# A fused mLSTM and two-MLP kernel in fp32: the order of the first three attention units, the weight swap two tiles earlier, and the last tile in thirds

## The reference, cut to what matters

```python
for t in range(S):                       # S = 768, 4 batches, 8 heads, head size 40
    m_new = np.maximum(f_gate[:, :, t] + m, i_gate[:, :, t])
    f_stab = np.exp(f_gate[:, :, t] + m - m_new)
    i_stab = np.exp(i_gate[:, :, t] - m_new)
    C = f_stab * C + i_stab * outer(v[t], k[t]);  n = f_stab * n + i_stab * k[t]
    y[:, :, t] = sigmoid(o_gate[t]) * (C @ q[t]) / np.maximum(np.abs(n @ q[t]), 1.0)
x = y as 3072 tokens x 320
h = x @ w_in;   x = np.maximum(0.01 * h, h) @ w_out      # MLP 1, 320 -> 2048 -> 320
h = x @ w2_in;  out = (h * np.cos(h)) @ w2_out           # MLP 2, same sizes
```

## Time and profile before

| | |
|---|---|
| median of 3 runs | 853.45 us (852.97 to 853.61) |
| profiled execution | 853.69 us, of which span 852.0 us |
| busy in the span: PE, DVE, ACT, POOL | 834.5, 626.1, 475.5, 311.9 us |
| DMA | 76.23 MB, 89 GB/s mean |

### The profile page before, as it was taken

The page is one execution under the profiler, slowest core; times in us unless marked ns, Lnnn a source line. Parts: engine busy times, 40 slices in busy tenths (PEclk is TensorE's granted clock), DMA queues, the critical chain, the costliest instruction groups (busy, mean ns, idle before and its releaser), DMA issues.

```text
span 852.0 us, 15386 instructions
## 1 busy us (share of the span) xinstructions
PE 834.5 (98%) x5618; PEld 820.9 (96%) x5618; DVE 626.1 (73%) x1175; ACT 475.5 (56%) x1041; POOL 311.9 (37%) x343
## 2 busy tenths in 40 slices
PE   7899999999999999999999989999999999999997
PEld 7789999999999999999999989999999999999997
DVE  6689777666676666776663478888888888888885
ACT  4355433433443434334335677777777777777775
POOL 4774533222222232432003663333333333333333
PEclk9899999999999999999999999999999999999999
DMA  8392822323433323225003430302010202020000
GB/s 261 102 299 73 279 91 90 136 90 100 151 132 112 136 90 136 90 90 203 2 27 120 135 110 1 117 1 70 1 71 1 70 1 71 0 70 2 15 10 23
DMA packets 38450, 76.23 MB, mean 89 GB/s; under 512 B 3434, under 2 KB 27498, under 8 KB 38378
## 3 DMA queue, kind: packets, MB, share of 16 engines
q1 hardware_dynamic: 38330, 75.23, 26.7%
q10 hardware_dynamic: 48, 0.05, 0.0%
HBM read 63.28 MB, written 11.99 MB: 88 GB/s over the span
## 4 chain that ended last, share of the span: by engine, by line
PE 58%; issue 23%; POOL 13%; DVE 2%; ACT 1%; DMA 1%; POOLq 0%; SPq 0%; ACTq 0%
PE h L574 22%; POOL g_lo L1283 13%; PE acc L584 7%; PE acc L586 7%; PE acc L585 7%; PE x L551 4%; PE s L497 3%; PE x L558 2%; PE x L539 1%; PE s L525 1%; PE s L574 1%; DMA kvo_s<-kvo 1%; PE acc L654 1%; DVE kvo_s L931 0%; DVE g_lo L1006 0%
## 5 line engine op out<-in xcount | busy, mean ns | idle before, releaser
L574 PE MATMUL h<-xT,w_in 128*128 128x384 f32 x1536 | 304.7, 340 | 1.3 <-DVE xT L998 1.3
L574 PEld LDWEIGHTS h<-xT,w_in 128*128 128x128 f32 x1536 | 268.4, 189 | 1.7 <-DVE xT L998 1.6
L700 ACT ACTIVATE t_f<-h 128x384 f32<-128x384 f32 x192 | 94.2, 490 | 296.0 <-PE h L574 296.0
L584 PE MATMUL acc<-w_out,g_hi 128*128 128x320 f32 x768 | 243.7, 317 | 4.6 <-POOL g_lo L1283 4.6
L586 PE MATMUL acc<-w_out,g_lo 128*128 128x320 f32 x768 | 237.4, 309 | 0.0
L585 PE MATMUL acc<-w_out,g_hi 128*128 128x320 f32 x768 | 236.1, 307 | 0.0
L1283 POOL TENSOR_TENSOR g_lo<-g_f,g_hi 128x384 fp32r<-128x384 f32 x128 | 131.7, 1029 | 213.6 <-ACT g_hi L700 213.6
L584 PEld LDWEIGHTS acc<-w_out,g_hi 128*128 128x128 f32 x768 | 144.4, 188 | 7.3 <-POOL g_lo L1283 3.1
L585 PEld LDWEIGHTS acc<-w_out,g_hi 128*128 128x128 f32 x768 | 144.5, 188 | 0.0
L586 PEld LDWEIGHTS acc<-w_out,g_lo 128*128 128x128 f32 x768 | 144.1, 188 | 0.0
L1013 DVE TENSOR_TENSOR g_f<-h,t_f 128x384 f32<-128x384 f32 x128 | 71.1, 555 | 96.7 <-ACT t_f L700 94.1
(11 more groups left out here) (134 smaller groups left out, 864.0 us busy)
## 6 DMA issues: line engine op xcount, KB each, us to landing
qk_s<-qk SPq DMA_DIRECT2D x24, 512.0 KB, 3.8
kvo_s<-kvo SPq DMA_DIRECT2D x24, 484.0 KB, 6.0
D<-g_dram SPq DMA_DIRECT2D x21, 512.0 KB
x_dram<-stage SPq DMA_DIRECT2D x8, 960.0 KB, 7.9
xT<-x_dram SPq DMA_DIRECT2D x8, 960.0 KB, 5.0
qe<-q SPq DMA_DIRECT2D x24, 180.0 KB, 4.0
out<-x SPq DMA_DIRECT2D x24, 160.0 KB, 1.8
raw_in<-w1i SPq DMA_DIRECT2D x8, 384.0 KB, 4.4
```

The source lines that it names most:

```text
L574: last = nc.tensor.matmul(bank[:, 0:BLOCK], w(a), x[:, k, :], start=(n == 0), stop=(n == 7))
L584: nc.tensor.matmul(acc[t][:, 0:DM], g_hi[:, s, r], w_out[:, 0, j, :], start=(j == 0), stop=False)
L700: copy = lambda o, i, **k: nc.scalar.activation(o, i, ACT.Copy, **k)
```

## The change

It touches the lists ahead of the first tile on all five engines, the place of one weight piece, the swap of the weights and the last tile. The core of the diff:

```diff
-LATE_IN = {0: 2, 2: 3, 5: 4, 7: 5, 9: 6, 11: 7}
+LATE_IN = {2: 2, 3: 3, 5: 4, 7: 5, 9: 6, 11: 7}
-SWAP_IN, SWAP_OUT = LAG, LAG + 1
+SWAP_IN, SWAP_OUT = 1, LAG + 1
-WARM = (9, 2, 3, 3, 4, 3)
+WARM = (10, 2, 5, 6)
...
             sp.wait_ge(G_done, 2)
             store_gates(g_dram, G_s[1].rearrange("p (c t) -> p c t", c=TILES), 1).then_inc(scratch, 16)
-            wait_count(xT_done, 1)
+            wait_count(x1_done, 1)
+            wait_count(U_done, 1)
             load_unit_inputs(0, 3)
             sp.wait_ge(gate_exp, 3)
             store_gates(e_dram, keep[:, TILES:CHUNKS, :], 1).then_inc(scratch, 16)
-            load_raw_in(w1i, 2)
             sp.wait_ge(scratch, 32)
             sp.wait_ge(g_stored, 16)
             load_unit_decays(0, 3)
+            load_raw_in(w1i, 2)
...
             warm_up(WARM[0], acc[0])
-            unit_scores(0, 0)
-            warm_up(WARM[1], acc[0])
             pe.wait_ge(sel_done, 2)
             pe.wait_ge(G_done, 1)
             spread_decays(0, 0)
             pe.wait_ge(i_step, 2)
             turn_columns(i_s, 0, 0)
             spread_decays(0, 1)
+            unit_scores(0, 0)
...
             spread_decays(1, 1)
+            spread_decays(2, 0)
             pe.wait_ge(cols_done, 2)
             unit_within(0, 0)
             unit_state(0, 0)
-            spread_decays(2, 0)
             spread_decays(2, 1)
-            warm_up(WARM[2], s_bank[1])
-            pe.wait_ge(dx_done, 2 * TILES)
             unit_scores(0, 2)
+            unit_state(0, 1)
+            pe.wait_ge(dx_done, 4)
             unit_carried(0, 1)
             unit_within(0, 1)
-            warm_up(WARM[3], s_bank[1])
+            pe.wait_ge(dx_done, 2 * TILES)
+            warm_up(WARM[1], acc[2])
             unit_transpose(0, 0)
-            unit_state(0, 1)
-            warm_up(WARM[4], h_bank[1])
             unit_carried(0, 2)
             unit_within(0, 2)
             unit_state(0, 2)
-            warm_up(WARM[3], h_bank[1])
             unit_transpose(0, 1)
-            warm_up(WARM[5], acc[2])
+            warm_up(WARM[2], acc[2])
             unit_transpose(0, 2)
+            warm_up(WARM[3], acc[2])
...
+            act.wait_ge(consts, 2)
+            copy(sel[:, :, :], ident[:, 0:HEADS].unsqueeze(2).to_broadcast([P, HEADS, CHUNK])).then_inc(sel_done, 1)
+            gate_scale(0)
             sigmoid_exp(0, 0)
-            gate_scale(0)
...
+            gate_maxima(1)
             sigmoid(0, 0)
-            gate_maxima(1)
             first_probs(0)
             sigmoid(0, 1)
-            first_probs(1)
+            first_probs(1, (0,))
+            gate_decays(1)
+            first_probs(1, (1,))
             outputs(0, 0)
-            first_probs(2)
+            first_probs(2, (0,))
+            sigmoid(0, 2)
+            first_probs(2, (1,))
             state(0, 1)
             outputs(0, 1)
-            gate_decays(1)
             x_lo(0, 0, xT[:, 0])
-            sigmoid(0, 2)
             outputs(0, 2)
...
+                if i >= 1 and ends(row, i - 1):
+                    last_cosines(row, i - 1)
...
+                elif ends(row, i):
+                    last_reduction(row, i, 0)
...
+                last_reduction(row, i, 1)
+                product(0)
+                last_reduction(row, i, 2)
+                rest(0)
+                product(1)
+                rest(1)
+                product(2)
+                rest(2)
```

More of the change, by code:

```diff
@@ L275, in swapped @@
             def swapped(self, i, after):
-                j = i - after
-                return j if self.starts(BLOCKS - 1, 0) and 0 <= j < FT else None
+                j = self.tile(i) - (BLOCKS - 1) * FT - after
+                return j if 0 <= j < FT else None
             def turn2(self, i):
@@ L304, in build, with ends, thirds @@
         TILES_TOTAL = 2 * BLOCKS * FT
+        def ends(row, i):
+            return isinstance(row.first, int) and row.tile(i) == TILES_TOTAL - 1
+        def thirds(x):
+            return [(c, x[:, c * P:(c + 1) * P]) for c in range(TILES)]
         def exists(row, i):
@@ L475, in score_banks @@
         def score_banks(b, c):
-            return (s_bank, h_bank, acc[1:3])[c] if first(b, c) else s_bank
+            return h_bank if first(b, c) and c == 1 else s_bank
         def output_bank(b, c):
@@ L481, in turn_bank @@
         def turn_bank(b, c):
-            return score_banks(b, c)[1] if first(b, c) else x_bank
+            return (acc[1], h_bank[1], s_bank[1])[c] if first(b, c) else x_bank
         @block.tensor
@@ L581, in second_product @@
                     r = slice(t * P, (t + 1) * P)
+                    if ends(row, i) and t > 0:
+                        pe.wait_ge(lo_done, row.tile(i) + 1 + t)
                     if j == 0:
@@ L760, in g_round, with last_cosines, cosine, rounded @@
                 copy(g_hi[:, i % RING, :], g_f[:, i % RING, :]).then_inc(hi_done, 1)
+            def last_cosines(row, i):
+                done = row.tile2(i) + 1
+                def cosine(c, r):
+                    act.wait_ge(red_done, done + T_FREE + c)
+                    nc.scalar.activation(r, r, ACT.Abs).then_inc(fold_done, 1)
+                    act.wait_ge(fold_done, done + c)
+                    nc.scalar.activation(r, r, ACT.Sin, bias=half_pi[:, 0:1], scale=-1.0).then_inc(sin_done, 1)
+                def rounded(c):
+                    act.wait_ge(prod_done, done + PROD_FREE + c)
+                    copy(g_hi[:, i % RING, c * P:(c + 1) * P], g_f[:, i % RING, c * P:(c + 1) * P]).then_inc(hi_done, 1)
+                for c, r in thirds(r_f[:, i % 2, :]):
+                    cosine(c, r)
+                    if c > 0:
+                        if c == 1:
+                            act.wait_ge(out_done, (row.tile(i) - RING + 1) * TILES + OUT_FREE)
+                        rounded(c - 1)
+                rounded(TILES - 1)
             def swap_in_hi(j):
@@ L798, in slot @@
                     g_round(row, i - 1)
-                if i >= 2 and exists(row, i - 2) and row.in_mlp2(i - 2):
+                if i >= 2 and exists(row, i - 2) and row.in_mlp2(i - 2) and not ends(row, i - 2):
                     act.wait_ge(prod_done, row.tile2(i) - 1 + PROD_FREE)
                     g_round(row, i - 2)
-                if i >= 1 and exists(row, i - 1) and row.in_mlp2(i - 1):
+                if i >= 1 and ends(row, i - 1):
+                    last_cosines(row, i - 1)
+                elif i >= 1 and exists(row, i - 1) and row.in_mlp2(i - 1):
                     r = r_f[:, (i - 1) % 2, :]
@@ L940, in probs, with first_probs @@
                 last.then_inc(P_done, 1)
-            def first_probs(c):
+            def first_probs(c, halves=(0, 1)):
                 dve.wait_ge(S_done, c + 1)
-                for e in range(2):
+                for e in halves:
                     dve.wait_ge(hm_done, 2 * c + e + 1)
@@ L1025, in slot @@
                     g_rest(row, i - 1)
-                if i >= 1 and exists(row, i - 1) and row.in_mlp2(i - 1):
+                if i >= 1 and ends(row, i - 1):
+                    last_products(row, i - 1)
+                elif i >= 1 and exists(row, i - 1) and row.in_mlp2(i - 1):
                     dve.wait_ge(sin_done, row.tile2(i))
@@ L1153, in first_columns, with first_mask @@
                 pool.wait_ge(colb_done, half + 1)
-            def first_mask(c):
-                for e in range(2):
+            def first_mask(c, halves=(0, 1)):
+                for e in halves:
                     pool.wait_ge(dx_done, 2 * c + e + 1)
@@ L1241, in split_out_lo @@
                                         w_out[:, 0, c, :].bitcast(F32), ALU.subtract).then_inc(wout_lo, 1)
+            second_rates()
             first_mask(0)
@@ L1291, in _ @@
                     swap_out_lo(i - SWAP_OUT)
-            with pool.Fori(1, BLOCKS) as n:
+            with pool.Fori(1, BLOCKS - 1) as n:
                 for s in range(FT):
                     g_rest(n * FT, s)
+            for s in range(FT - 1):
+                g_rest((BLOCKS - 1) * FT, s)
 def kernel(q, k, v, i_gate, f_gate, o_gate, moe_w_in, moe_w_out, moe2_w_in, moe2_w_out):
```

62 lines of the change are left out of this document (42 added, 20 removed).

## The result

The changed kernel takes 844.79 us (median of 4 runs, 844.61 to 846.09), the one before in the same rounds 853.53 us (852.97 to 853.88): a ratio of 0.9892, 95% interval 0.9872 to 0.9911. The prediction was 845.2. The profiled execution took 844.61 us with a span of 842.9, against 853.69 and 852.0: 9.1 us of span are gone.

What follows compares the result with a forecast made beforehand. Chain through all engines bounds it before 40 us, PE alone from 58 to 500, ACT, DVE and POOL at two places. 5.6 + 1.6 + 1.1 = 8.3 off 853.69 gives 845.4, as median 845.2 us; range 842.3 to 848.2.

Steps and rivals of the forecast that it cites:

- The first tile: First MLP tile on PE: start at 35.5 instead of 40.08, 4.6 us earlier, a shift kept by everything behind it.
- First decays: Start of the chain: with spreads ahead of scores, ACT's column copy comes at 10.3 instead of 13.14, 2.8 us earlier.
- The stretch to the first tile: From third unit's carried part to first tile: 9.1 us before; 6.9 at full clock, 8.4 if it falls, 7.7 taken.
- The qe product behind the mask: POOL ahead of the third unit's carried part: qe product now follows the mask, making the gain 3.5 us instead of 4.6.
- The first block's slots: First tile to fourth unit's state: faster first products worth 1.5 us, 1.0 counted because DVE limits; bounds 0 and 3.0.
- The fourth unit's early loads: Fourth unit's inputs and decays asked for some ten microseconds before POOL needs them; counted as nothing.
- The change to MLP 2: PE's g_lo waits of 1.28 and 1.02 us: the first goes, 0.7 of the second stays; gain 1.6, bounds 1.0 and 2.3.
- The last tile: End of the kernel: last tile in 128-column pieces, 0.29 us each on ACT, ends at 847.9, 1.1 us earlier.
- Rival A: Before the first tile: low clock, late scores or DVE's list cut its gain to 2 to 3 us; 848.3 us; 15%.
- B: Rival: clock does not fall and PE's 1.51 us wait in the slots goes; gain 11.5, time 842.0; 15%.
- E: Rival: PE's clock falls before the third unit's carried part, stays low in the first block's slots; 857 after four; 4%.
- signs of being wrong: First tile later than 37.5, a new PE wait between 58 and 490 us, or ACT pieces above 0.4 us each.

Runs made afterwards that it cites:

- w_state: Changed kernel with the second unit's state on DVE put ahead of the third unit's reciprocal and second half of its probabilities; 842.22 us, ratio 0.9879.
- u_fill: Changed kernel with seven warm-up products more in PE's pause behind the turning of the first unit; 842.41 us, ratio 0.9849.
- x_scan: u_scores with one wait added: POOL holds the second unit's qe product until DVE's scan of the second half's decays is done; 846.60 us, ratio 0.9914.
- u_scores: Changed kernel with the first unit's scores and two warm-up products put back ahead of the spreads on PE; 849.20 us, ratio 0.9938.
- v_qe: Changed kernel with the third unit's qe product put ahead of the second masked state on POOL; 840.71 us, ratio 0.9829.
- u_swap: Changed kernel with the swap of the input weights back at its old place (`SWAP_IN = LAG`); 848.11 us, ratio 0.9920.
- u_whole: Changed kernel with the last tile kept in one piece, as before the change; 846.75 us, ratio 0.9903.
- w_both: Changed kernel with the edits of w_state and v_qe together and two warm-up products fewer; 839.54 us, ratio 0.9832.
- v_again: The changed kernel itself, run once more unaltered; 845.24 us, ratio 0.9882.
- v_nowarm: Changed kernel without the six warm-up products right ahead of the first tile (`WARM[3]` set to 0); 845.59 us, ratio 0.9889.

## Why the prediction was right, step by step

The sum was 8.3 us and the span lost 9.1, the median 8.7. Sign, range and the forecast's own range held. Its terms:

- **The first tile, 4.6 predicted, 4.7 measured.** The number was right by luck, by two errors against each other. *First decays*: "Column copy at 10.3" was 9.05, 4.1 earlier instead of 2.8. The exponential ahead of the copy started at 8.63 instead of 9.83: the input that ACT's sigmoid waits for let it start at 7.75 instead of 8.54, 0.8 sooner, and `gate_scale(0)`, now ahead of the sigmoid, took its own exponential out from behind that wait, 0.4. The prediction held both fixed. The input's part is chance to some degree: in the changed kernel and the twelve others this sigmoid starts anywhere from 7.33 to 8.19. The third unit's scores came at 17.98, below 19.7 to 20.9, and the carried part at 25.75, not 27.5. *The stretch to the first tile* was to be 7.7 and was 9.6: the clock was low for 7 of them, more than the 3 us of before on which the prediction's 8.4 for that case rests. At full clock the stretch takes 6.4 (24.29 to 30.68 in w_state, 27.72 to 34.11 in u_fill), against the 6.9 worked out, so the clock cost 3.2 us here, where 1.5 was allowed.
- **What the step did not contain.** DVE's scan of the second half's decays was moved and counted at nothing. x_scan and u_scores show that its place decides over 3.2 us. Before, it already took 1.91 beside POOL's split of w_in; in the changed kernel it falls into a wait of POOL. By an estimate from x_scan's 3.2, the first tile would have come near 38.6 had the scan fallen beside such a row.
- **The qe product behind the mask, 1.1, measured 1.1** (v_qe), with some 1.6 to 2.0 more at the first tile, through the clock in that one profile, which the prediction had not tied to it.
- **The first block's slots, 1.0 predicted, 2.1 measured**, inside its bounds of 0 and 3.0. The eight products took 1.66 where 2.93 were taken before, 1.3 by the clock; the column turn within them was 0.2 shorter; PE's wait for DVE fell from 1.51 to 0.97, 0.5. The step that failed is "then waits for the second one; I count 1.0 of the 1.5": counted from the first tile the state came 2.1 sooner, so DVE passed on nearly all. `LATE_IN`, whose term was nothing ("DVE's sum is unchanged there"), gained 0.3. The fourth unit's early loads count nothing: right (0.1).
- **The change to MLP 2, 1.6 predicted, 1.8 measured** in the waits and 1.7 by u_swap. The second wait kept 0.32, not 0.7.
- **The last tile, 1.1 predicted, 0.3 to 0.4 measured** (u_whole). From the g_hi of the tile before the last to the last product it is 4.98 us instead of 5.14, only 0.2 less. The step that failed is the size "in between 0.29" for all nine pieces: the absolute value and the rounding take 0.29 to 0.31, the sine 0.40, which adds 0.3; and ACT waited 0.38 and 0.56 for DVE, 0.4 more than the 0.5 allowed. "No trace row has the pieces of 128 columns on ACT" was not so either: the eight exponentials of 128 columns at 21.41 took 2.15, 0.27 each; the sine of 128 columns alone had no row. The third that was to free DVE early, ahead of the g_hi, took 1.02 beside POOL's g_lo instead of 0.29, so the g_hi stands only 0.1 earlier than in u_whole (785.12 against 785.26 behind the state) and not 0.3. The measured gain lies nearer to the bound of zero than to the forecast.

The rule of the Trainium skill ("VectorE: DVE Perf Modes", The TRN2 errata), a fixed cost for each instruction, spoke against the thirds. Three thirds of DVE's product take 3 x 0.29, against 0.55 for the whole (833.23 in u_whole), so the trace agrees in kind that three small pieces cost more than one whole. It did not turn the sign. The prediction's loss of "0.1 or so" by that rule has no working behind it, and the copy of 64 columns that it set beside the rule reads from PSUM (acc), not from SBUF as the rule wants.

Rival A's mechanism, a clock that falls and stays low until the first tile, happened by half in the profiled run: it fell at 26 and was back at 33, ahead of the first tile and its slots, and its price was paid out of a larger gain. B's, no fall of the clock, is seen in w_state. E did not happen: in the profiles of the changed kernel and the twelve others, windows of 1 us from the first tile to 60 us show no clock below 0.95. Of the signs of being wrong, none came in the changed kernel's profile (the sine's 0.40 stands at the limit), but u_swap, with the same list up to there, had its first tile at 38.02, beyond the 37.5 named: the sign would have depended on the execution.

**What stays open.** Why the low stretch begins at 23 in one execution and at 28 in another, and lasts 3 to 14 us, with one and the same list in front of it. What part of the first tile's gain against the kernel before is the order and what part the clock of that execution, in a single profile of each, stays open with it. A shorter pause of PE went with a higher mean clock in v_qe and in four of five executions of w_both, but not in the fifth, nor in two of the four of w_state.

## What to carry to other kernels

Price a moved instruction by what runs beside it at its new place, on the other engine too: a DVE scan of 0.93 us took 4.16 beside POOL's row, and a wait added to POOL brought the first tile forward by 3.2 us. Where PE must pause before a critical row of products, see what clock the row behind it was granted before believing a sum made at full clock, and try a shorter pause (v_qe) or a filled one (u_fill); neither makes the clock certain. Profile one list more than once before a microsecond at one place is called the effect of an edit. A tail cut in pieces gains less than its pieces promise when another engine's whole-size work still runs beside them: here a third took 1.02 us instead of 0.29.

## What the hardware did that I had not expected

- DVE's TENSOR_TENSOR_SCAN of 32x384 took 0.91 to 1.01 with POOL idle, 1.13 beside the end of a mask, 1.91 beside one POOL product of 1.81 (the kernel before, at 31.53), and 4.16 beside a row of POOL instructions, ending with the last of them (at 21.71 and 21.83). The prediction used the rule of the Trainium skill ("SBUF — State Buffer", Who interferes with whom) for one g_lo alone; these rows agree with it, and x_scan shows the effect by taking the neighbour away.
- The granted clock differed between executions of one list. Those seven kernels had the low stretch at 26 to 33, 23 to 33, 23 to 37, 29 to 32, 25 to 35, 28 to 34 and 28 to 35 us, and the first tile between 34.24 and 38.02 (v_nowarm's, at 37.01, without the last six products). In v_again the part of it that lay beside PE's pause cost nothing.
